# Expert stage: gathered rows transposed by VectorE instead of TensorE, and gathered three tiles ahead

## The chip, the cores and the metric

One Trainium2 chip, one core. The metric is the device time of one execution in microseconds (us), median over runs. Engines: PE is TensorE, DVE VectorE, ACT ScalarE, POOL GpSimd, SP SyncE.

## What is computed

Three layers follow one another: linear attention on 8 x 8 heads of 576 positions, a gated dense layer, and a layer of 8 experts. In the reference, cut to what matters here (N = 4608 tokens, D = 512, F = 1024, E = 8):

```python
logits = x @ w_gate
expert_idx = np.argmax(logits, axis=1)
gate_w = softmax(logits)[np.arange(N), expert_idx]
for e in range(E):
    mask = expert_idx == e
    xe = x[mask]
    h = np.maximum(xe @ w1[e], 0.0)
    ye = h @ w2[e]
    out[mask] = gate_w[mask, None] * ye
```

## The kernel before

The program is written engine by engine; each engine runs its own list in order, with waits on semaphores. A fp32 operand of a matmul is kept as two parts, `hi` (rounded) and `lo` (the rest), and a product is the sum of three matmuls (`split3`). So each operand costs a cast (ScalarE) and a subtraction (VectorE).

The expert stage works on tiles of 128 tokens of one expert. With these inputs there are 40 tiles, g = 0 to 39. Tiles 0 to 2 (`FIRST` = 3) and the last are written out; tiles 3 to 38 are a loop on every engine (`tiles`), whose bounds and addresses come from a table in memory (`table`). One pass of the loop for tile g is, engine by engine:

- PE (`tile`, L1763): `first_product(g)`, two halves of 12 matmuls of 512 columns; `x_transpose(g + 1)`, four transposes of 128 x 128 from the gathered rows `xg` into the PSUM bank `xtr_ps` (L1715); `second_product(g - 2)`, 24 matmuls.
- ACT (L1288): `relu_stored(g)` from PSUM to `hs` (L1257); `rows_high(g + 1)`, the cast from `xtr_ps` to the high half of `xt` (L1232); `next_gate` (L1242); `turned_h_high(g - 1)`, the cast of `hturn` to the high half of `ht` (L1286); then the casts of the weight chunks that the table gives to this tile (L810).
- DVE (L1504): `rows_low(g + 1)`, the subtraction from `xtr_ps` for the low half of `xt` (L1463); `turn_h(g - 1)`, one transpose of 128 x 1024 in blocks of 32 x 32 from `hq` to `hturn` (L1489); `result(g - 2)`, PSUM to `ysb` (L1470); `turned_h_low(g - 1)`, the subtraction for the low half of `ht` (L1494); the subtractions of the weight chunks (L1501).
- POOL (`period`): `gather(g + 2)`, an indirect DMA of 128 rows of 513 numbers into `xg` (L1086), with the gate of the tile before saved first (L1077); `scatter(g - 2)`, an indirect DMA of `ysb` to the output (L1109).
- SP (L1025): `store_rows(g)`, h to memory; `load_quarters(g)`, h back into `hq` with its quarters exchanged, so that 32 x 32 blocks complete its transpose; `loads_of(g - 1)`, loads of weight chunks of 1 MB into four slots (`ahead`).

An expert's weights are four chunks of 128 x 2048. They lie split in `ring`, which holds two experts; the table says at which tile each chunk is cast.

`hturn` is the low half of `ht`, so `turn_h(g - 1)` waits for the end of the second product of the tile before, and `turned_h_low` subtracts in place. There is one `xt` buffer, one `xg`, one `hq` and one `ysb`. In the loop `xt` is written between two first products:

```python
def x_transpose(g):
    pe.wait_ge(gathered, 16 * g + 16)
    for c in range(DC):
        last = pe.transpose(xtr_ps[:, c * P:(c + 1) * P], xg[:, c * P:(c + 1) * P], m["ident"][:])
    last.then_inc(xtr_mm, 1)
```

Of the kernel before, what the change touches and what calls it, by code (L numbers as in the profile page):

```python
# [22 lines left out]
F32 = mybir.dt.float32  # L23
# [43 lines left out]
def alloc(nc, ctx):  # L67
# [58 lines left out]
    for name, n, dt in (("ident", P, F32), ("tri", P, F32), ("ones", P, F32),   # L126
                        ("wgate", DC * E, F32), ("absmax", 8 * PT, F32), ("cden", H * S // DK, F32),
                        ("ibase", BQ * E, F32), ("idesc", BQ * E, F32),
                        ("cum", (BQ + 1) * E, F32), ("rt", 4 * BQ * E, F32), ("lg", BQ * E, F32), ("rq", 6 * BQ, F32),
                        ("slot", BQ, U32), ("tokf", BQ, F32),  # L130
                        ("ids0f", FIRST, F32), ("ids0", FIRST, U32), ("pad", 2, F32),
                        ("idall", 3 * P, U32), ("idg", 1, U32), ("ids", 1, U32),
                        ("gate", 1, F32), ("gnext", 1, F32), ("tabf", 5 * GMAX, F32), ("tab", 5 * GMAX, I32),
                        ("thr", E * TPE, F32), ("gi", GMAX * E, F32), ("nte", 4 * E, F32),
                        ("lowtri", E * E, F32)):
        m[name] = sb(name, [P, n], dt)
# [690 lines left out]
def stage2(nc, m, t):  # L827

    with ExitStack() as ctx:
# [18 lines left out]
        h_turned, gate_saved = sem("s3_h_turned"), sem("s3_gate_saved")  # L848
        h_stored, hq_in = sem("s3_h_stored"), sem("s3_hq_in")
# [195 lines left out]
        def _(pool):  # L1045
# [43 lines left out]
            def gather(g):  # L1089
                if isinstance(g, int):  # L1090
                    pool.wait_ge(gate_set, g)
                    pool.wait_ge(xtr_mm, g)
                    ids_of(g)
                else:
                    keep_gate(g - 1)
                    ids_of(g)
                    pool.wait_ge(gate_saved, g)
                    pool.wait_ge(xtr_mm, g)
                gather_rows(g)
# [39 lines left out]
            gather(FIRST + 1)  # L1139
            pool.wait_ge(y_sb, 2)  # L1140
# [4 lines left out]
            def period(g):  # L1145
                gather(g + 2)
                scatter(g - 2)

            last = tiles(pool, period, 2)
# [15 lines left out]
        def _(act):  # L1165
# [71 lines left out]

            def next_gate(g):
                for h in range(2):
                    act.wait_ge(relu_done[h], g)  # L1240
                act.wait_ge(gate_saved, g + 1)
                act.copy(m["gate"][:], m["gnext"][:]).then_inc(gate_set, 1)  # L1242
# [45 lines left out]
            def tile(g):  # L1288
                relu_stored(g)
                rows_high(g + 1, False)  # L1290
                next_gate(g + 1)
                turned_h_high(g - 1)
                tile_chunks(act, g, weights)
# [28 lines left out]
        def _(dve):  # L1322
# [142 lines left out]

            def result(g):
# [37 lines left out]
            def tile(g):  # L1504
                rows_low(g + 1)
                turn_h(g - 1)
                result(g - 2)
                turned_h_low(g - 1)
                tile_chunks(dve, g, weights)

            dve.sem_inc(h_turned, 2)
            turns(dve, turn)
# [44 lines left out]
            dve.tensor_copy(m["idall"][:], last_ps[:, 0:3 * P]).then_inc(idt_sb, 1)  # L1557
# [49 lines left out]
            linked(dve.tensor_scalar_add(tabf[:, 3, 4:5], tabf[:, 3, 0:1], -4.0), base)  # L1607
            dve.tensor_copy(m["tab"][:, 0:ROW], m["tabf"][:, 0:ROW]).then_inc(tabs, 1)
# [8 lines left out]
            weights(CPE)  # L1617
            weights(CPE + 1)
            last = tiles(dve, tile)
            last1 = last_of(dve, 1)  # L1620
# [10 lines left out]
        def _(pe):  # L1631
# [131 lines left out]
            def tile(g):  # L1763
# [3 lines left out]
                x_transpose(g + 1)  # L1767
# [90 lines left out]
```

## Time and profile before

| | |
|---|---|
| median of 3 runs | 1505.48 us (1502.93 to 1506.18) |
| the profiled execution | 1503.65 us, span of its core 1501.9 us |
| TensorE busy | 1470.3 us |
| VectorE busy | 877.1 us |
| ScalarE busy | 620.6 us |
| GpSimd busy | 527.4 us |
| granted TensorE clock | 0.995 of full speed |

The last third of the span, from about 1040 us on, is the loop over tiles and its end. How to read the rows: in a timeline each row has the start in us from the span's start, the length in us, the engine, the line of the kernel, the operation, what it writes and reads, how many were merged, and in brackets how long the engine had been idle before it and what ended that. Lines are those of the kernel before; L167 is the helper that records every split matmul.

### The profile page before, as it was taken

The numbers are of one execution on the slowest core, as the hardware profiler recorded it, in microseconds if no ns is written. First come the engines' busy times: TensorE is split into PE (matmuls) and PEld (weight loads), VectorE is DVE, ScalarE is ACT, GpSimd is POOL, SyncE is SP. The second block draws the span as 40 slices with busy tenths as digits, with TensorE's granted clock in tenths as the row PEclk, the third lists the DMA queues.
The fourth block names the chain that finished last, engine by engine and source line by source line (L and its number), as shares of the span: only waits on it lengthen the run. The fifth ranks groups of instructions, "written<-read, shape, count | busy, mean of one in ns | idle before, by whom it ended". The sixth has DMA issues, their size and how long they took to land.

```text
span 1501.9 us, 29607 instructions
## 1 busy us (share of the span) xinstructions
PE 1470.3 (98%) x8062; PEld 1272.5 (85%) x8063; DVE 877.1 (58%) x1629; ACT 620.6 (41%) x1295; POOL 527.4 (35%) x653
## 2 busy tenths in 40 slices
PE   7999999999989999999999999999999999999996
PEld 6999999999978888888888888888888778888885
DVE  4688888888825473746547274635555545553332
ACT  5688788788822122221212222133344334442221
POOL 6676677676820020120202022030344333332321
PEclk9999999999999999999999999999999999999999
DMA  7354344444440112020211202065676767653441
GB/s 259 111 140 102 103 112 102 111 104 114 120 129 0 41 44 83 1 84 4 79 35 49 78 6 84 2 152 147 217 233 221 236 211 230 229 193 132 140 142 40
DMA packets 111242, 173.49 MB, mean 116 GB/s; under 512 B 52976, under 2 KB 72176, under 8 KB 106978
## 3 DMA queue, kind: packets, MB, share of 16 engines
q1 hardware_dynamic: 103618, 152.82, 34.2%
q0 software_dynamic: 7584, 20.17, 4.0%
q8 instruction: 21, 0.34, 0.1%
q14 instruction: 19, 0.16, 0.0%
HBM read 123.66 MB, written 50.34 MB: 116 GB/s over the span
## 4 chain that ended last, share of the span: by engine, by line
PE 68%; DMA 1%; issue 1%; DVE 1%; SPq 0%; ACT 0%; ACTq 0%; POOL 0%; POOLq 0%; DVEq 0%
PE bank L167 66%; PE bank L1715 1%; DMA h_scratch<-arena 0%; DMA arena<-we 0%; DMA arena<-rows_scratch,idg 0%; PE bank L1646 0%; SPq L1022 0%; DMA arena<-h_scratch 0%; PE bank L1759 0%; DVE hturn L1489 0%; DVE big L1501 0%; PE bank L1654 0%; PE bank L1665 0%; ACT big L810 0%; PE bank L1640 0%
## 5 line engine op out<-in xcount | busy, mean ns | idle before, releaser
L167 PE MATMUL bank<-big,xs 128*128 (+1 forms) x2100 | 493.5, 393 | 13.2 <-DVE big L610 8.1
L167 PEld LDWEIGHTS bank<-big,xs 128*128 128x128 f32 x2100 | 392.4, 189 | 95.2 <-issue 14.7
L167 PE MATMUL bank<-xs,big 128*128 128x512 f32 x1728 | 397.4, 391 | 2.7 <-PEq L216 2.7
L167 PEld LDWEIGHTS bank<-xs,big 128*128 128x128 f32 x1728 | 324.7, 188 | 70.4 <-issue 3.0
L167 PE MATMUL bank<-big 128*128 128x512 f32 (+1 forms) x1632 | 325.9, 348 | 2.0 <-POOL big L306 1.4
L167 PEld LDWEIGHTS bank<-big 128*128 128x128 f32 (+1 forms) x1632 | 255.9, 165 | 36.2 <-POOL big L306 1.7
L1050 POOL TENSOR_TENSOR arena<-arena 128x512 f32<-128x512 f32 x32 | 41.0, 1293 | 438.2 <-DMA arena<-rec_scratch 438.2
L1432 DVE TENSOR_TENSOR arena<-arena,bank 128x512 f32<-128x512 f32 x72 | 49.5, 687 | 243.9 <-PE bank L167 243.9
L1189 ACT COPY arena<-bank 128x512 f32<-128x512 f32 x72 | 42.4, 589 | 307.0 <-PE bank L167 307.0
L1357 DVE CUSTOM_DVE_ANT_0 arena<-arena 128x512 f32<-128x512 f32 x256 | 159.6, 689 | 16.1 <-ACT arena L1209 15.4
L704 PE MATMUL bank<-arena 128*128 128x66 f32 (+1 forms) x1152 | 147.8, 269 | 0.0
L704 PEld LDWEIGHTS bank<-arena 128*128 128x128 f32 x1152 | 142.3, 191 | 0.2
L1109 POOL DMA_INDIRECT out<-arena,ids x38 | 69.0, 1815 | 209.1 <-DVE arena L1470 202.1
L181 POOL TENSOR_TENSOR kqs<-kqraw,kqs 128x256 fp32r<-128x256 f32 (+1 forms) x160 | 128.2, 801 | 12.8
L508 ACT ACTIVATE arena<-arena 128x256 f32<-128x256 f32 (+1 forms) x320 | 110.4, 399 | 50.9 <-DVE arena L634 40.8
L167 PE MATMUL bank<-wphis,kqs 128*128 128x256 f32 x864 | 130.8, 290 | 0.3
L1286 ACT CAST xs<-hturn 128x1024 fp32r<-128x1024 f32 x37 | 39.0, 1053 | 191.2 <-DVE hturn L1489 191.2
L622 DVE TENSOR_REDUCE absmax<-bank 128x4 f32<-128x512 f32 (+1 forms) x160 | 100.7, 630 | 22.2 <-PE bank L167 21.6
L634 DVE TENSOR_TENSOR arena<-bank,absmax 128x512 f32<-128x512 f32 (+1 forms) x160 | 102.2, 639 | 18.0
L167 PEld LDWEIGHTS bank<-wphis,kqs 128*128 128x128 f32 x864 | 111.3, 189 | 1.7 <-DVE arena L634 1.5
L1489 DVE STREAM_TRANSPOSE hturn<-arena 128x1024 f32<-128x1024 f32 x37 | 46.1, 1245 | 106.1 <-PE bank L167 96.7
L1501 DVE TENSOR_TENSOR big<-arena,big (+1 forms) x28 | 64.1, 2295 | 52.4 <-ACT big L810 52.4
(182 smaller groups left out, 1350.6 us busy)
## 6 DMA issues: line engine op xcount, KB each, us to landing
arena<-we SPq DMA_DIRECT2D x32, 1024.0 KB, 11.5
h_scratch<-arena SPq DMA_DIRECT2D x37, 512.0 KB
arena<-h_scratch SPq DMA_DIRECT2D x148, 128.0 KB
kqraw<-kq SPq DMA_DIRECT2D x32, 576.0 KB, 3.8
rows_scratch<-arena SPq DMA_DIRECT2D x36, 256.5 KB
xT_scratch<-arena SPq DMA_DIRECT2D x32, 288.0 KB
arena<-v SPq DMA_DIRECT2D x64, 128.0 KB, 2.4
arena<-xT_scratch SPq DMA_DIRECT2D x8, 1024.0 KB, 5.2
```

Source lines behind the costliest of these rows:

```text
L167: ins = nc.tensor.matmul(out, left[a], right[b], start=first and n == 0, stop=last and n == 2)
L181: pool.tensor_tensor(m["kqs"][:, 1, u, cols], m["kqraw"][:, u, cols], m["kqs"][:, 0, u, cols].bitcast(F32), ALU.subtract).then_inc(m["kq_l ...
L508: last = act.activation(ke[:, rows[0]:rows[-1] + 1, s * P:(s + 1) * P], pm[:, rows[0]:rows[-1] + 1, 0], ACT.Exp, scale=1.0 - 2.0 * s)
L622: dve.tensor_reduce(absmax[:, bank, 0:n], proj_ps[bank][:, 0:2 * n * P].rearrange("p (t a f) -> p t a f", t=n, a=2), AX.X, ALU.max, apply_ ...
L634: dve.tensor_tensor(pm[:, rows[0]:rows[-1] + 1], proj_ps[bank][:, 0:2 * n * P].rearrange("p (t a f) -> p t a f", t=n, a=2), absmax[:, bank ...
L704: last = pe.matmul(kv_ps[:, s, cols[0]:cols[1]], ke[:, r, s * P:(s + 1) * P], v[:, u, slots[0]:slots[1]].rearrange("p t d -> p (t d)"), st ...
L1109: pool.indirect_dma_start(t["out"], bass.IndirectOffsetOnAxis(m["ids"][:, 0:1], 0), ysb, None, bounds_check=N - 1, oob_is_err=False).then_ ...
L1189: act.copy(asb[:, j % 2], a_ps[j % 2][:]).then_inc(a_sb, 1)
L1357: dve.tensor_tensor_reduce(products[e % 2], x2[:, q, 0:DM], m["wgrows"][:, e * DM:(e + 1) * DM], 1.0, 0.0, ALU.mult, ALU.add, lg[:, n:n + ...
L1432: dve.tensor_tensor(abf[:, j % 2], asb[:, j % 2], b_ps[j % 2][:], ALU.mult).then_inc(ab_f, 1)
L1489: dve.transpose(m["hturn"].rearrange("p (k b j) -> p k b j", k=FC, b=P // Q), hq.rearrange("p (b k i) -> p k b i", b=P // Q, k=FC)).then_i ...
L1501: dve.tensor_tensor(ring[:, 1, ds(at, CW)], ahead[:, ds(slot, CW)], ring[:, 0, ds(at, CW)].bitcast(F32), ALU.subtract).then_inc(w_lo, 1)
```

## The change

The transposes of the gathered rows leave TensorE from tile 4 on. VectorE does them instead (`turn_rows`), from `xg` to a new buffer `xturn`. Its transpose works on blocks of 32 x 32 within 32 partitions, so 128 x 128 is put together from sixteen instructions a tile: for each quarter a of the partitions written and each quarter b of those read, one transposes four blocks, 32 partitions by 128 elements. The cast and the subtraction for `xt` then read `xturn` instead of PSUM (`turned_rows_high`, `turned_rows_low`).

`turn_rows(g + 2)` stands in VectorE's pass for tile g, after the subtraction for tile g + 1 and ahead of `turn_h(g - 1)`. `xg` is free when it is done, so GpSimd's gather runs three tiles ahead instead of two, and waits for VectorE (`x_turned`) instead of TensorE. Ahead of the loop, VectorE turns tile 4 between the two weight chunks that stand there, and GpSimd gathers tile 5. The end of the loop is written out for one tile more on VectorE and GpSimd, the table gets one more entry, and the list of tokens `idall` is cut to the 288 columns in use.

```diff
+                        ("xturn", DM, F32), ("idall", E * TPE + 4, U32), ("idg", 1, U32), ("ids", 1, U32),
...
             def gather(g):
-                if isinstance(g, int):
+                if isinstance(g, int) and g <= FIRST + 1:
                     pool.wait_ge(gate_set, g)
                     pool.wait_ge(xtr_mm, g)
                     ids_of(g)
@@
                     keep_gate(g - 1)
                     ids_of(g)
                     pool.wait_ge(gate_saved, g)
-                    pool.wait_ge(xtr_mm, g)
+                    pool.wait_ge(x_turned, g)
                 gather_rows(g)
@@
             gather(FIRST)
             gather(FIRST + 1)
+            gather(FIRST + 2)
...
             def period(g):
-                gather(g + 2)
+                gather(g + 3)
                 scatter(g - 2)
@@
+            def turned_rows_high(g):
+                act.wait_ge(x_turned, g + 1)
+                act.wait_ge(h_mm, 2 * g)
+                act.copy(m["xt"][:, 0], m["xturn"][:]).then_inc(xt_hi, 1)
@@
             def tile(g):
                 relu_stored(g)
-                rows_high(g + 1, False)
+                turned_rows_high(g + 1)
                 next_gate(g + 1)
                 turned_h_high(g - 1)
                 tile_chunks(act, g, weights)
@@
+            def turn_rows(g):
+
+                dve.wait_ge(xt_lo, g)
+                dve.wait_ge(gathered, 16 * g + 16)
+                by_token = xg[:, 0:DM].rearrange("p (c a j) -> p a c j", c=DC, a=P // Q)
+                by_row = m["xturn"][:].rearrange("p (c b i) -> p b c i", c=DC, b=P // Q)
+                for a in range(P // Q):
+                    for b in range(P // Q):
+                        last = dve.transpose(by_row[a * Q:(a + 1) * Q, b], by_token[b * Q:(b + 1) * Q, a])
+                last.then_inc(x_turned, 1)
+
+            def turned_rows_low(g):
+                dve.wait_ge(xt_hi, g + 1)
+                dve.wait_ge(h_mm, 2 * g)
+                dve.tensor_tensor(m["xt"][:, 1], m["xturn"][:], m["xt"][:, 0].bitcast(F32), ALU.subtract
+                                  ).then_inc(xt_lo, 1)
@@
             def tile(g):
-                rows_low(g + 1)
+                turned_rows_low(g + 1)
+                turn_rows(g + 2)
                 turn_h(g - 1)
                 result(g - 2)
                 turned_h_low(g - 1)
                 tile_chunks(dve, g, weights)
 
             dve.sem_inc(h_turned, 2)
+            dve.sem_inc(x_turned, FIRST + 1)
...
             weights(CPE)
+            turn_rows(FIRST + 1)
             weights(CPE + 1)
-            last = tiles(dve, tile)
-            last1 = last_of(dve, 1)
+            last = tiles(dve, tile, 2)
...
@@
                 for h in range(2):
                     first_product(g, h, *here)
-                x_transpose(g + 1)
                 second_product(g - 2, *before)
```

How the instructions of the loop stand on VectorE, from the instruction ahead of the loop to the first half of a pass. `arena` is the memory that holds `xg`, `hq` and `ysb`; `xs` holds `xt` and `ht`; `big` is `ring`. Before:

```order
L1501 TENSOR_TENSOR big<-arena,big 128x2048 x2
L824 TENSOR_LOAD tab
L824 ISA x2
L915 UNCONDITIONAL_BRANCH
L915 ISA
L1463 TENSOR_TENSOR xs<-bank,xs 128x512
L1487 ISA
L1489 STREAM_TRANSPOSE hturn<-arena 128x1024
L1469 ISA
L1470 COPY arena<-bank 128x512
L1493 ISA
L1494 TENSOR_TENSOR xs<-hturn,xs 128x1024
```

And in the change:

```order
L1482 STREAM_TRANSPOSE xturn<-arena 32x4x32 x16
L1526 TENSOR_TENSOR big<-arena,big 128x2048
L824 TENSOR_LOAD tab
L824 ISA x2
L916 UNCONDITIONAL_BRANCH
L916 ISA
L1487 ISA
L1488 TENSOR_TENSOR xs<-xturn,xs 128x512
L1477 ISA
L1482 STREAM_TRANSPOSE xturn<-arena 32x4x32 x16
L1512 ISA
L1514 STREAM_TRANSPOSE hturn<-arena 128x1024
```

Sixteen transposes stand between the subtraction for `xt` and the transpose of h in each pass, with no wait among them (ISA rows are waits and register work), and another sixteen between the two weight chunks ahead of the loop.

On TensorE, between the first and the second product of a pass. Before:

```order
L167 MATMUL bank<-big,xs 128x512 x2
L1713 ISA
L1715 MATMUL bank<-ident,arena 128x128 x4
L1732 REGISTER_ALU
L1737 ISA
```

And in the change:

```order
L167 MATMUL bank<-big,xs 128x512
L167 ISA
L167 MATMUL bank<-big,xs 128x512 x2
L1766 REGISTER_ALU
L1771 ISA
```

The four transposes and their wait for the gather are gone; the second product follows the first at once.

## Rows read from the trace of the kernel before

**Rows 1.** The page's table of engines: busy us, share of the span, instructions

```profile
PE 1470.3 (98%) x8062; PEld 1272.5 (85%) x8063; DVE 877.1 (58%) x1629; ACT 620.6 (41%) x1295; POOL 527.4 (35%) x653
```

**Rows 2.** The chain of waits in the loop: start us, us, what

```profile
1302.36 0.44 PE bank L1715 x4
1302.80 10.92 PE bank L167 x48
```

**Rows 3.** Groups of instructions on TensorE, whole span: busy us, mean ns, idle before

```profile
L1715 PE MATMUL bank<-ident,arena 128*128 128x128 f32 x160 | 24.0, 273 | 0.1
```

**Rows 4.** VectorE's timeline, one tile with one chunk

```profile
1297.03 1.25 DVE L1489 STREAM_TRANSPOSE hturn<-arena 128x1024 f32<-128x1024 f32 x1 [3.11 <-PE bank L167]
...
1299.51 1.23 DVE L1494 TENSOR_TENSOR xs<-hturn,xs 128x1024 fp32r<-128x1024 f32 x1 [0.67 <-ACT xs L1286]
...
1302.38 2.29 DVE L1501 TENSOR_TENSOR big<-arena,big  x1 [1.64 <-ACT big L810]
...
1304.59 0.68 DVE L1463 TENSOR_TENSOR xs<-bank,xs 128x512 fp32r<-128x512 f32 x1
...
1308.38 1.25 DVE L1489 STREAM_TRANSPOSE hturn<-arena 128x1024 f32<-128x1024 f32 x1 [3.10 <-PE bank L167]
```

**Rows 5.** Groups of instructions on VectorE, 1060 to 1475 us

```profile
L1494 DVE TENSOR_TENSOR xs<-hturn,xs 128x1024 fp32r<-128x1024 f32 x36 | 44.1, 1226 | 24.0 <-ACT xs L1286 24.0
L1463 DVE TENSOR_TENSOR xs<-bank,xs 128x512 fp32r<-128x512 f32 x36 | 24.7, 687 | 39.5 <-ACT xs L1232 38.8 <-issue 0.7
```

**Rows 6.** VectorE's timeline, two instructions with no wait between

```profile
1033.48 0.28 DVE L1547 TENSOR_SCALAR arena<-arena,rq 128x128 f32<-128x128 f32 x1
1033.67 0.43 DVE L1548 TENSOR_SCALAR arena<-arena,rq 128x288 f32<-128x288 f32 x1
```

**Rows 7.** VectorE's timeline, the two memsets of 64 partitions

```profile
2.44 0.17 DVE L594 MEMSET arena<- 64x132 f32 x1
2.69 0.17 DVE L595 MEMSET arena<- 64x132 f32 x1
```

**Rows 8.** VectorE's timeline, two instructions linked by a semaphore

```profile
1047.82 0.15 DVE L1604 TENSOR_SCALAR tabf<-tabf 128x1 f32<-128x1 f32 x1
1048.01 0.15 DVE L1605 TENSOR_SCALAR tabf<-tabf 128x1 f32<-128x1 f32 x1
```

**Rows 9.** ScalarE's timeline in the same tile as rows 4

```profile
1298.36 1.05 ACT L1286 CAST xs<-hturn 128x1024 fp32r<-128x1024 f32 x1 [5.71 <-DVE hturn L1489]
...
1300.08 1.91 ACT L810 CAST big<-arena  x1 [0.67 <-issue]
...
1301.89 1.26 ACT L1257 ACTIVATE arena<-bank,gate 128x512 f32<-128x512 f32 x2
```

**Rows 10.** Groups of instructions on VectorE, 1060 to 1475 us: the weight chunks

```profile
L1501 DVE TENSOR_TENSOR big<-arena,big x26 | 59.6, 2296 | 52.4 <-ACT big L810 52.4
```

**Rows 11.** VectorE's timeline, first transpose of h, and first after the last chunk

```profile
1064.55 1.25 DVE L1489 STREAM_TRANSPOSE hturn<-arena 128x1024 f32<-128x1024 f32 x1 [3.82 <-PE bank L167]
...
1365.20 1.25 DVE L1489 STREAM_TRANSPOSE hturn<-arena 128x1024 f32<-128x1024 f32 x1 [3.11 <-PE bank L167]
```

**Rows 12.** A tile without a chunk: a piece of the chain, and VectorE's timeline

```profile
1381.90 0.44 PE bank L1715 x4
...
1383.43 0.69 DVE L1463 TENSOR_TENSOR xs<-bank,xs 128x512 fp32r<-128x512 f32 x1 [3.16 <-ACT xs L1232]
```

**Rows 13.** Ahead of the loop: a piece of the chain, and timelines

```profile
1045.16 3.60 DMA arena<-rows_scratch,idg
...
1051.74 0.97 POOL L1086 DMA_INDIRECT arena<-rows_scratch,idg  x1 [0.83 <-DVE arena L1470]
...
1053.74 4.48 DVE L1501 TENSOR_TENSOR big<-arena,big 128x2048 fp32r<-128x2048 f32 x2
...
1057.36 0.91 POOL L1077 COPY gnext<-arena 128x1 f32<-128x1 f32 x1 [3.30 <-DMA arena<-rows_scratch,idg]
```

**Rows 14.** VectorE's timeline, a chunk in one of the first ten tiles

```profile
1105.16 2.29 DVE L1501 TENSOR_TENSOR big<-arena,big  x1 [2.82 <-ACT big L810]
```

More of the change, by code:

```diff
@@ L131, in alloc @@
                         ("ids0f", FIRST, F32), ("ids0", FIRST, U32), ("pad", 2, F32),
-                        ("idall", 3 * P, U32), ("idg", 1, U32), ("ids", 1, U32),
+                        ("xturn", DM, F32), ("idall", E * TPE + 4, U32), ("idg", 1, U32), ("ids", 1, U32),
                         ("gate", 1, F32), ("gnext", 1, F32), ("tabf", 5 * GMAX, F32), ("tab", 5 * GMAX, I32),
@@ L848, in stage2 @@
         h_turned, gate_saved = sem("s3_h_turned"), sem("s3_gate_saved")
+        x_turned = sem("s3_x_turned")
         h_stored, hq_in = sem("s3_h_stored"), sem("s3_hq_in")
@@ L1145, in period @@
             def period(g):
-                gather(g + 2)
+                gather(g + 3)
                 scatter(g - 2)
-            last = tiles(pool, period, 2)
+            last = tiles(pool, period, 3)
+            scatter(last_of(pool, 4))
             keep_gate(last)
@@ L1556, in _ @@
             dve.wait_ge(idt_mm, 1)
-            dve.tensor_copy(m["idall"][:], last_ps[:, 0:3 * P]).then_inc(idt_sb, 1)
+            dve.tensor_copy(m["idall"][:, 0:E * TPE], last_ps[:, 0:E * TPE]).then_inc(idt_sb, 1)
             linked(dve.tensor_tensor(gw, gi, ends.unsqueeze(1).to_broadcast([P, GMAX, E]), ALU.is_ge), base)
@@ L1607, in _ @@
             linked(dve.tensor_scalar_add(tabf[:, 3, 4:5], tabf[:, 3, 0:1], -4.0), base)
+            linked(dve.tensor_scalar_add(tabf[:, 3, 5:6], tabf[:, 3, 0:1], -5.0), base)
             dve.tensor_copy(m["tab"][:, 0:ROW], m["tabf"][:, 0:ROW]).then_inc(tabs, 1)
@@ L1617, in _ @@
             weights(CPE)
+            turn_rows(FIRST + 1)
             weights(CPE + 1)
-            last = tiles(dve, tile)
-            last1 = last_of(dve, 1)
+            last = tiles(dve, tile, 2)
+            last1, last2 = last_of(dve, 1), last_of(dve, 2)
+            turned_rows_low(last)
+            turn_h(last2)
+            result(last_of(dve, 3))
+            turned_h_low(last2)
+            tile_chunks(dve, last1, weights)
             last_low()
```

## The prediction

> **What bounds the kernel now.** I read the page's table of engines first: TensorE is busy for 98% of the span, VectorE for 58% [rows 1]. Then the chain of waits in the expert stage: it is TensorE alone, 10.93 us for 48 matmuls, then 0.44 us for the four transposes of the gathered rows, 11.37 us a tile [rows 2]. So the transposes lie on the path. The groups of instructions give their number: 160 records for 40 tiles, 24.0 us busy, 0.15 us each when overlapped [rows 3]; four of the 40 sets (tiles 0 to 3) stay. Last I read VectorE's timeline of one tile, since the work goes there [rows 4]: transpose of h (1297.03), result copy, subtraction for `ht`, weight chunk (1302.38), subtraction for `xt` (1304.59), and then 3.10 us of waiting for TensorE before the next transpose of h at 1308.38. That idle time is all that VectorE can take on in such a tile before it sets the pace.
>
> **What goes.** 36 sets of transposes on TensorE, 36 x 0.44 = 15.8 us of the chain. If TensorE stayed the bound everywhere, that would be the result: about 1488 us. ScalarE's and VectorE's `xt` steps read SBUF in place of PSUM; VectorE takes 1226 ns for 1024 columns from SBUF and 687 ns for 512 from PSUM [rows 5], one price per column, so I cost this at nothing; the reads stand on the path only where VectorE does, and are counted there.
>
> **What comes: sixteen transposes a tile on VectorE.** One covers 32 partitions and 128 elements each. Its length: the rows of 512 and 1024 columns differ by 539 ns, 1.05 ns a column [rows 5]; the transpose of 1024 columns takes 1.25 us [rows 4], so 0.17 us is fixed, and 128 columns take 0.17 + 0.13 = 0.30 to 0.31 us. What decides is the distance from one start to the next, and the trace of before has no such series. Its bounds:
> - Below: two instructions with no wait between, all on partitions from 0 up, overlap. The compare of 128 columns at 1033.48 lasts 0.28 us and the next starts 0.19 us after it [rows 6]. At 0.19 to 0.20 us sixteen take 3.0 to 3.2 us.
> - Above: the only pair without a wait whose partitions change is that of the two memsets of 64 rows (partitions 64 to 127, then 0 to 63). They do not overlap: 0.17 us long, 0.25 us apart [rows 7], 0.08 us from end to start. At 0.31 + 0.08 = 0.39 us sixteen take 6.2 us.
> - Between: where each instruction waits for the one before by a semaphore, the start comes 0.04 us after the end (0.15 us long, 0.19 apart) [rows 8].
>
> In the change the quarter that is read differs from one transpose to the next in all sixteen, so the memsets are the nearest pair: I take no overlap. For the gap I take the 0.04 us of instructions that read, since a memset reads nothing: 0.31 + 0.04 = 0.35 us, R = 5.6 us a tile. Bounds 5.0 (no gap) to 6.2.
>
> The memsets show a change of the partitions written, not of those read. Taken that narrowly, only the four transposes that begin a new output quarter would be serial, and the sum 1522 (third rival). The Trainium skill, "VectorE: DVE Perf Modes", section on two Vector instructions with no wait between them, says that one is held until all earlier ones have finished when its first input or its output starts in another group of 32 partitions than the last. By it all sixteen are held and the sum is the one below, 1571. No row here shows a changed input alone. The same page, section on the three transpose paths, gives 311 ns for a VectorE transpose of 128 columns and says that it stays within 32 x 32 blocks, so TensorE is its choice for a full one; by its figure the sixteen would be an estimated 5.0 us plus gaps.
>
> **A tile with one weight chunk.** VectorE's own chain: from the transpose of h to the chunk 5.35 us (1297.03 to 1302.38), chunk to `xt` subtraction 2.21, that one 0.68 and 0.04 to the sixteen, which wait for it, then R, then the next transpose of h [rows 4]. The 5.35 us can't shrink, because the chunk's cast on ScalarE (1300.08, 1.91 us) stands behind its cast of the turned h (1298.36) [rows 9]. Sum 8.28 + 5.6 = 13.88 us, against 11.35 now. TensorE needs 10.93 and idles 2.9 us in each.
>
> Queued behind the sixteen on VectorE: `turn_h`, `result`, `turned_h_low`, the chunk. The second product waits for `turned_h_low`, SyncE's quarter loads and weight loads for `turn_h`, GpSimd's scatter for `result`. These come late together and stay in the same order; the scatter and the loads have the longer tile to finish in.
>
> **The run of tiles.** In the loop there are 26 chunks [rows 10]; the timeline has them as 10 tiles with one, one with two, one with none, 14 with one, then 10 tiles with none. From the first transpose of h in the loop to the first after the last chunk now: 1064.55 to 1365.20, 300.65 us for 26 tiles [rows 11]. Changed: 24 x 13.88 = 333.1. The tile with two chunks takes one more 2.2: 16.1. The one without: ScalarE's cast of the turned h ends 2.4 us after the transpose of h began; then it has its table loads, two activations (1.26 us together) and the cast for `xt` [rows 9], so I estimate that the `xt` subtraction starts at 5.4, and the tile takes 5.4 + 0.7 + 5.6 = 11.7. Sum 360.9: **+60.3 us**.
>
> **The start.** VectorE turns tile 4 between two chunks ahead of the loop. Now the two run together, 4.48 us from 1053.74; the rows of tile 4 are gathered from 1051.74 on and are there at 1057.36, when GpSimd's copy that waited for them starts [rows 13]. So turning is 1057.4 to 1063.0, the chunk to 1065.2, the `xt` subtraction to 1065.9. The gather for tile 5 now waits for the first turning: from about 1063.1, with 3.6 us (the gather at 1045.16 was in the chain for that long) to 5.6 us, to 1066.7; turning to 1072.3. The transpose of h stood at 1064.55: **+7.7**.
>
> **The end.** At the last chunk TensorE is no longer 5.9 us from its next second product when `turn_h` starts, but 3.7, since the first product is done: **-2.2**. In the ten tiles without chunks the `xt` subtraction starts 1.5 us after the first product's end (1383.43, and the chain goes over to the transposes at 1381.90) [rows 12]; 1.5 + 0.7 + 5.6 + 3.7 (transpose of h to the end of the `ht` subtraction [rows 4]) = 11.5 where TensorE wants it at 10.93. A second product that starts 0.6 late gives the next tile as much room, so they take 11.2 on average, against 11.37: **-1.5**.
>
> **First ten tiles.** There ScalarE reaches its chunk up to 1 us later (VectorE waits 2.82 us for it at 1105.16, against 1.64 at 1302.38 [rows 4, 14]), while DMA is fullest. Now TensorE hides it, then nothing would: 0 to +10. DMA has a fifth more time in the longer tile; I take **+3**.
>
> **Sum:** 60.3 + 7.7 - 2.2 - 1.5 + 3 = +67.3. The profiled execution took 1503.65 us (span 1501.9), inside the runs' 1502.93 to 1506.18 and 1.8 below their median. Forecast **1571 us**. The 15.8 us are all given back, and four times as much again.
>
> **Range of this case.** R = 5.0 is 0.6 x 26 = 16 less and 2 less at the start and the end; with nothing for the first ten tiles 1550. R = 6.2 gives 16 more and 4 at the start and the end; with the whole +10, 1598. A gather that is late would also be dear: issued at the end of one turning, it is needed 13.88 - 5.6 = 8.3 us later, and takes 3.6 to 5.6 [rows 13]; at 9 it would add 0.7 x 26 = 18 us, 1589. Range 1549 to 1600, a step beyond both ends.
>
> **Rivals.**
> 1. *The transposes overlap* (faster, 8%). Place: the same sixteen instructions. The point from which it decides is a pitch of (11.35 - 8.28) / 16 = 0.19 us, and the compares show just that. Against: the memsets, and the compares never move between partitions. At 0.19: R = 3.0, a tile with a chunk takes 11.3 as now; the last ten are TensorE's at 10.93, 4.4 less; the waits of TensorE about the tile with two chunks shrink by at most 2: **1497**. At 0.20 to 0.21, or with the first ten tiles' cost, it is a tie.
> 2. *TensorE stays the bound in all tiles* (faster, 1%): 1488. It needs R below 10.93 - 8.28 = 2.65, a pitch of 0.17.
> 3. *Only a new output quarter is serial* (slower, 7%). Four at 0.35 and twelve at 0.20: R = 3.8, a tile 12.08: 24 x 0.73 = 17.5 more; start +4, first ten +3, the end -2.2 - 4.4: **1522**. For it: the memsets show no more. Against: nothing shows an input moved without cost.
> 4. *Serial, as forecast* (slower, 84%).
>
> A change within 0.2% (3 us, about what can be told from none) lies about a pitch of 0.19 to 0.20. Of the first rival's 8%, 4 are faster by more than that, 3 the tie, 1 slower. Faster 4 + 1 = 5%, same 3%, slower 84 + 7 + 1 = 92%. The range of the forecast's own case holds nearly all of its 84%, so it stands.
>
> **What would show it.** In the changed profile: transposes of `xturn` with starts 0.35 us apart and 5.6 us in all; the group of L1715's transposes with 16 records; tiles of 13.9 us between transposes of h up to the last chunk, with TensorE waiting 2.9 us ahead of each second product for the `ht` subtraction; tiles of about 11.2 after it; the chain of waits on VectorE for most of the expert stage. Starts 0.2 us apart would make it wrong at the root; starts 0.35 apart with tiles near 11.4 would mean that the 5.35 us before the chunk shrinks after all.

## The result, and the profile after

The changed kernel took **1562.82 us** (median of 4 runs, 1559.56 to 1563.42), the kernel before 1505.83 on the same chip (4 runs, 1502.93 to 1507.56): a ratio of 1.0376, interval 1.0354 to 1.0398. The forecast was 1571, range 1549 to 1600. The profiled execution took 1563.42 us, span 1561.7, so the span grew by 59.8 us.

The page's table of engines for the changed kernel:

```profile
PE 1481.9 (95%) x7918; PEld 1270.4 (81%) x7919; DVE 1057.2 (68%) x2206; ACT 619.6 (40%) x1295; POOL 497.9 (32%) x653
```

TensorE has 144 matmuls fewer than in [rows 1], 36 sets of four, and is nevertheless busy 11.6 us longer (the last section returns to this). VectorE has 577 instructions and 180.1 us more, of which the page's group of transposes holds 576 and 174.5 us (busy us, mean ns; then idle time ahead):

```profile
L1482 DVE STREAM_TRANSPOSE xturn<-arena 32x128 f32<-32x128 f32 x576 | 174.5, 303 | 16.3 <-DMA arena<-rows_scratch,idg 4.2
```

The chain of waits in the same stage, at the start of one set of sixteen (start us, us, what):

```profile
1313.48 0.30 DVE xturn L1482
1313.79 0.01 issue
1313.80 0.30 DVE xturn L1482
...
1314.11 0.30 DVE xturn L1482
1314.41 0.01 issue
1314.42 0.30 DVE xturn L1482
```

Starts 0.31 us apart, 0.01 us from end to start, one strictly after the other. And they stand in the chain, where [rows 2] had nothing but TensorE. VectorE's timeline of one tile with a chunk, to be laid beside [rows 4]:

```profile
1332.05 1.25 DVE L1514 STREAM_TRANSPOSE hturn<-arena 128x1024 f32<-128x1024 f32 x1
1333.22 0.65 DVE L1495 COPY arena<-bank 128x512 f32<-128x512 f32 x1
1334.54 1.22 DVE L1519 TENSOR_TENSOR xs<-hturn,xs 128x1024 fp32r<-128x1024 f32 x1 [0.66 <-ACT xs L1294]
1337.41 2.29 DVE L1526 TENSOR_TENSOR big<-arena,big  x1 [1.65 <-ACT big L810]
1339.62 0.68 DVE L1488 TENSOR_TENSOR xs<-xturn,xs 128x512 fp32r<-128x512 f32 x1
1340.44 5.05 DVE L1482 STREAM_TRANSPOSE xturn<-arena 32x128 f32<-32x128 f32 x16
1345.53 1.25 DVE L1514 STREAM_TRANSPOSE hturn<-arena 128x1024 f32<-128x1024 f32 x1
```

The 3.1 us in which VectorE waited for TensorE are gone. 5.36 us from the transpose of h to the chunk, as before; the sixteen take 5.09 us up to the next transpose of h; the tile 13.48. TensorE's timeline around the same place:

```profile
1322.48 11.19 PE L167 MATMUL bank<-big,xs 128*128 x48 [0.69 <-DVE xs L1519]
1335.96 12.77 PE L167 MATMUL bank<-big,xs 128*128 x48 [2.29 <-DVE xs L1519]
1349.44 11.17 PE L167 MATMUL bank<-big,xs 128*128 x48 [0.70 <-DVE xs L1519]
```

Each row is a tile's second product and the first product behind it. So in every tile TensorE now waits ahead of the second product for VectorE's subtraction for `ht`, 0.7 and 2.3 us by turns. Where the span's 59.8 us lie:

| stretch | before, us | after, us | difference | forecast |
|---|---|---|---|---|
| up to the first transpose of h in the loop | 1064.55 | 1073.55 | +9.0 | +7.7 |
| from there to the first one after the last chunk | 300.65 | 352.84 | +52.2 | +63.3 |
| the rest | 136.7 | 135.3 | -1.4 | -3.7 |

The rows are those of one execution. The first stretch differs from one to the next: in *swapped* below, with the same sixteen instructions there, it ends at 1069.66, since the first turning finds its rows already there. The stretch ends so (VectorE's timeline of the changed kernel):

```profile
1057.87 5.05 DVE L1482 STREAM_TRANSPOSE xturn<-arena 32x128 f32<-32x128 f32 x16 [1.55 <-DMA arena<-rows_scratch,idg]
1062.95 2.29 DVE L1526 TENSOR_TENSOR big<-arena,big 128x2048 fp32r<-128x2048 f32 x1
1065.16 0.68 DVE L1488 TENSOR_TENSOR xs<-xturn,xs 128x512 fp32r<-128x512 f32 x1
1068.47 5.05 DVE L1482 STREAM_TRANSPOSE xturn<-arena 32x128 f32<-32x128 f32 x16 [2.63 <-DMA arena<-rows_scratch,idg]
1073.55 1.25 DVE L1514 STREAM_TRANSPOSE hturn<-arena 128x1024 f32<-128x1024 f32 x1
```

and one of the last ten tiles, without a chunk, looks so: VectorE,

```profile
1460.53 1.25 DVE L1514 STREAM_TRANSPOSE hturn<-arena 128x1024 f32<-128x1024 f32 x1
...
1466.00 0.69 DVE L1488 TENSOR_TENSOR xs<-xturn,xs 128x512 fp32r<-128x512 f32 x1 [1.75 <-ACT xs L1244]
1466.84 5.05 DVE L1482 STREAM_TRANSPOSE xturn<-arena 32x128 f32<-32x128 f32 x16
1471.92 1.25 DVE L1514 STREAM_TRANSPOSE hturn<-arena 128x1024 f32<-128x1024 f32 x1
```

and ScalarE:

```profile
1461.87 1.05 ACT L1294 CAST xs<-hturn 128x1024 fp32r<-128x1024 f32 x1 [7.29 <-DVE hturn L1514]
1463.79 1.27 ACT L1265 ACTIVATE arena<-bank,gate 128x512 f32<-128x512 f32 x2 [0.87 <-issue]
1465.24 0.62 ACT L1244 CAST xs<-xturn 128x512 fp32r<-128x512 f32 x1 [0.18 <-ACT arena L1265]
```

Here TensorE sets nothing. The tile is a loop of VectorE and ScalarE: transpose of h, its cast, the table loads (0.87), two activations, the cast for `xt`, its subtraction (5.47 us after the transpose of h began), the sixteen. It takes 11.39 us, as long as the tile before the change. Eight of the ten tiles are such, 11.36 to 11.40. The ninth takes 9.77: its pass has no rows left to turn. That tile, 1.6 us shorter than before, is the -1.4 of the table's last line; the tenth takes 11.80, before 11.81.

### The profile page after: what moved, and what is told of

The parts are those of the page before. It is cut to its first block and busy times, and to the rows that moved or that the text cites. A ratio compares the mean times of both kernels' runs of the same rounds, so it can differ in the third digit from the quotient of the medians.

```text
span 1561.7 us, 29935 instructions
## 1 busy us (share of the span) xinstructions
PE 1481.9 (95%) x7918; PEld 1270.4 (81%) x7919; DVE 1057.2 (68%) x2206; ACT 619.6 (40%) x1295; POOL 497.9 (32%) x653
## 5 line engine op out<-in xcount | busy, mean ns | idle before, releaser
L167 PE MATMUL bank<-big,xs 128*128 (+1 forms) x2100 | 510.7, 403 | 61.9 <-DVE xs L1519 50.2
L167 PEld LDWEIGHTS bank<-big,xs 128*128 128x128 f32 x2100 | 405.7, 195 | 162.4 <-issue 77.8
L1482 DVE STREAM_TRANSPOSE xturn<-arena 32x128 f32<-32x128 f32 x576 | 174.5, 303 | 16.3 <-DMA arena<-rows_scratch,idg 4.2
L1087 POOL DMA_INDIRECT arena<-rows_scratch,idg x37 | 38.1, 1030 | 203.9 <-DVE xturn L1482 202.2
L1526 DVE TENSOR_TENSOR big<-arena,big (+1 forms) x28 | 64.1, 2292 | 43.6 <-ACT big L810 43.6
## 6 DMA issues: line engine op xcount, KB each, us to landing
arena<-we SPq DMA_DIRECT2D x32, 1024.0 KB, 11.7
```

The lines of the kernel that those rows point to most:

```text
L167: ins = nc.tensor.matmul(out, left[a], right[b], start=first and n == 0, stop=last and n == 2)
L1482: last = dve.transpose(by_row[a * Q:(a + 1) * Q, b], by_token[b * Q:(b + 1) * Q, a])
L1526: dve.tensor_tensor(ring[:, 1, ds(at, CW)], ahead[:, ds(slot, CW)], ring[:, 0, ds(at, CW)].bitcast(F32), ALU.subtract).then_inc(w_lo, 1)
```

## Experiments

All change the changed kernel, by the diff shown. A single run's time is set beside the kernel before on the same chip: 1506.51 us for the first four, 1502.93 for *late*, *behind_chunk* and *moved*, 1505.07 for *late_scatter* and *behind_scatter*, 1504.14 for *moved_act*, 1505.28 for *chunk_first*. "Tile" is the distance between transposes of h in tiles with one chunk.

### What sets the pitch of the sixteen

**same_quarter.** Each transpose reads the quarter that it writes, so 12 of 16 change neither (its blocks off the diagonal are other data than the reference's).

```diff
-                        last = dve.transpose(by_row[a * Q:(a + 1) * Q, b], by_token[b * Q:(b + 1) * Q, a])
+                        last = dve.transpose(by_row[a * Q:(a + 1) * Q, b], by_token[a * Q:(a + 1) * Q, b])
```

> The sixteen transposes stay, but in each group of four both the quarter read and the quarter written stay the same (the turned rows are then not the transposed ones: blocks outside the diagonal are wrong, so h and the output are). Theory (a transpose waits for the end of the one before only when its partitions move): inside a group the starts are 0.19 to 0.21 us apart, between groups 0.32; R = 12 x 0.20 + 4 x 0.32 = 3.7 us, a tile with a chunk 8.40 + 3.7 = 12.1 us, the time about 1518 us. Rival (transposes never overlap, wherever they read and write): all starts 0.32 apart, R = 5.1, 13.5 us a tile, 1562 us.

Measured 1517.67 us, tile 12.0. The chain of waits shows groups of four:

```profile
1309.00 0.88 DVE xturn L1482 x4
1309.88 0.01 issue
1309.89 0.88 DVE xturn L1482 x4
```

Within a group there are three pitches of 0.19 us and one whole instruction; between groups there is a gap of 0.01 us and no overlap. The same sixteen instructions of the same size take 3.6 us instead of 5.08. The pitch is a matter of quarters, not of the transpose.

**swapped.** The loops over a and b exchange places: 12 of 16 change only the quarter written, where the changed kernel has 12 that change only the quarter read.

```diff
-                for a in range(P // Q):
-                    for b in range(P // Q):
+                for b in range(P // Q):
+                    for a in range(P // Q):
```

> The two loops exchanged: the quarter written changes with each transpose, the quarter read with every fourth. Nothing else changes. Theory (a change of either is enough): starts 0.32 us apart, 1562 us within 3. Rival (only one of the two counts, and the other's cost is what the changed kernel paid): starts 0.20 apart inside a group, about 1518 us.

Measured 1558.66 us (one run, 3.3 below the 1562 expected; it comes to the loop's first transpose of h 3.9 us sooner than the changed kernel), tile 13.47, starts 0.31 to 0.32 apart. Either change, of the quarter read or of the one written, holds the instruction. With the changed kernel's own rows this ends the third rival.

**twelve and eight.** Fewer transposes: `for a in range(3)` and `for a in range(2)`. The rest of `xturn` is zero, so a quarter or a half of each gathered row's transpose is left out.

```diff
-                for a in range(P // Q):
+                for a in range(3):
@@
-            dve.sem_inc(x_turned, FIRST + 1)
+            dve.memset(m["xturn"][:], 0.0).then_inc(x_turned, 1)
+            dve.wait_ge(x_turned, 1)
+            dve.sem_inc(x_turned, FIRST)
```

> Twelve of the sixteen transposes, the last quarter of xturn left at zero (a quarter of the contraction is left out in tiles from 4 on). Theory (VectorE's own chain, 8.40 us and the transposes, sets the tile): R = 3.8, a tile with a chunk 12.2 us, tiles without one 10.93, the time 1562.8 - 26 x 1.27 - 2.5 - 4.4 = about 1523 us. Rival (the gather, which now waits for VectorE and takes some 5.5 us to land, or GpSimd's queue sets it): less than half of that is won, over 1540.

> Eight of the sixteen, half of xturn left at zero (half of the contraction is left out in tiles from 4 on). Theory: R = 2.5, 8.40 + 2.5 = 10.9, so TensorE sets the pace again at 10.93 us a tile and the whole gain of its lost transposes shows, but for the start: about 1489 us. Rival (a slow TensorE clock after each wait, or the gather, keeps tiles at 11.2 or more): 1497 or more.

Twelve: 1527.25 us, tile 12.3, most of the last ten 10.88. Eight: 1497.25 us, tile 10.93 in most from the seventh on. Four transposes are worth 1.2 us a tile while VectorE sets the pace, and with eight the pace is TensorE's. Both came out longer than expected. Twelve missed by 4 us, in two tiles: 13.62 near the start and 15.2 behind the tile without a chunk. Eight missed by 8 us and came out at its rival's 1497, but not for the rival's reason: its usual tile is 10.93 and not 11.2, and the granted clock fell only once in the loop. Its first six tiles take 11.2 to 11.9, since ScalarE comes late to its chunk there (3 us in all), and the three tiles about the one with two chunks take 13.36, 9.74 and 15.76, 6 us more than three of 10.93. In the longest of them ScalarE's activations wait 5.22 us for the store of h.

### Where the sixteen stand

VectorE still waits 0.66 + 1.65 us a tile for ScalarE ahead of the `ht` subtraction and the chunk. Could the sixteen fill that?

**late.** Behind the `ht` subtraction, ahead of the chunk.

```diff
             def tile(g):
                 turned_rows_low(g + 1)
-                turn_rows(g + 2)
                 turn_h(g - 1)
                 result(g - 2)
                 turned_h_low(g - 1)
+                turn_rows(g + 2)
                 tile_chunks(dve, g, weights)
```

> turn_rows(g + 2) moved behind turned_h_low(g - 1), ahead of the weight chunk, where VectorE now idles 1.65 us for ScalarE's cast. Theory (VectorE's chain is its work plus its waits for ScalarE, and work put into a wait is free): from the transpose of h 3.75 us to the sixteen, 5.08, the chunk 2.21, the xt subtraction 0.60: 11.7 us a tile with a chunk, the tiles without one 10.9, the start 7 us earlier; about 1505 us in all, no change against the kernel before. Rival (VectorE is simply 5.1 us fuller, wherever they stand, or the gather behind them comes late): 13.4 us a tile, over 1550.

Measured **1626.23 us** (1620.84 to 1630.37), ratio 1.0804 (1.0772 to 1.0837). The theory fell. VectorE's timeline, then GpSimd's:

```profile
1342.92 0.69 DVE L1495 COPY arena<-bank 128x512 f32<-128x512 f32 x1 [3.24 <-DMA out<-arena,ids]
...
1344.66 5.04 DVE L1482 STREAM_TRANSPOSE xturn<-arena 32x128 f32<-32x128 f32 x16
```

```profile
1350.69 2.80 POOL L1087 DMA_INDIRECT arena<-rows_scratch,idg  x1 [8.75 <-DVE xturn L1482]
...
1354.66 1.03 POOL L1110 DMA_INDIRECT out<-arena,ids  x1 [0.97 <-POOL ids L1106]
```

GpSimd's queue has the scatter behind the gather three tiles ahead, and that gather waits for the sixteen. Turned later, they hold the gather, the gather holds the scatter, and the next result copy on VectorE waits for the scatter that frees `ysb`: 3.24 us here. I had counted who waits for the sixteen, and not who stands behind the one that waits.

**behind_chunk.** Behind the chunk too, last in the pass.

```diff
                 turned_h_low(g - 1)
                 tile_chunks(dve, g, weights)
+                turn_rows(g + 2)
```

> The sixteen behind the weight chunk, so no longer ahead of turn_h and the ht subtraction, but not in a wait either. Theory (what counts is the sum round the loop): 8.3 + 5.1 = 13.4 us a tile with a chunk, about 1555 us. Rival (the harm is that the transposes delay turn_h and with it the second product; anywhere behind it they are free): about 11.4 us a tile, 1505 us.

Measured 1681.12 us, one run, most tiles 16.9 to 17.8; in one of them the result copy waits 5.51 us for the scatter.

**late_scatter and behind_scatter.** The same two, with GpSimd's scatter ahead of its gather.

```diff
             def period(g):
-                gather(g + 3)
                 scatter(g - 2)
+                gather(g + 3)
```

> The run with the sixteen ahead of the chunk again, with GpSimd's scatter(g - 2) now ahead of its gather(g + 3). Theory (in that run the scatter stood behind a gather that waited for the sixteen, and VectorE's result copy waited for the scatter, a circle of two engines; and of VectorE's 1.65 us ahead of the chunk about 1 us is its own table loads, which only a wait can hide): the result copy waits no more, 3.75 + 5.08 + 1.05 + 2.21 + 0.6 = 12.7 us a tile with a chunk, 10.9 without, about 1533 us. Rival (the gather that comes late is what costs): the tiles stay at 14 us or more, over 1570.

> The run with the sixteen behind the chunk again, with the scatter ahead of the gather. Theory (sum round VectorE's loop): 5.35 + 2.21 + 5.08, then 0.87 of waiting for ScalarE's cast of the turned rows, which can now start only behind the sixteen, and 0.60: 14.1 us a tile with a chunk, about 1570 us. Rival (harm only ahead of turn_h): 11.4 us a tile, 1505.

late_scatter: **1536.14 us** (1534.84 to 1546.15), ratio 1.0228 (1.0193 to 1.0263), tile 12.1 in most after the first five. The whole came out near what was expected (1533), but its parts didn't: the tile was to be 12.7, of which the table loads ahead of the chunk took 0.6 instead of 1.05, and the first five tiles took 13.0 to 14.7. behind_scatter: 1570.11 us, one run, tile 14.10. One exchange of two calls on GpSimd takes 90 and 111 us off, so the loop through the scatter is shown. It also shows what the place is worth: ahead of the chunk the sixteen run while ScalarE casts it, the tile is 1.4 us shorter than the changed kernel's 13.47 and the whole 27 us; behind the chunk there is no wait to fill, and a new one comes: the `xt` subtraction waits 0.87 us for ScalarE's cast of rows that were turned only just before.

**moved.** GpSimd copies the gathered rows to a second buffer `xh` as soon as they and the last turning are done, so the next gather waits for that copy and not for VectorE. Two transposes stand ahead of the `ht` subtraction, fourteen ahead of the chunk.

```diff
+            def move_rows(g):
+                pool.wait_ge(x_turned, g)
+                pool.sem_inc(turn_taken, 1)
+                pool.tensor_copy(m["xh"], xg[:, 0:DM]).then_inc(x_moved, 1)
@@
-                    pool.wait_ge(x_turned, g)
+                    move_rows(g - 1)
+                    pool.wait_ge(x_moved, g)
@@
                 turned_rows_low(g + 1)
-                turn_rows(g + 2)
                 turn_h(g - 1)
                 result(g - 2)
+                turn_rows(g + 2, 0, 2)
                 turned_h_low(g - 1)
+                turn_rows(g + 2, 2, 16)
                 tile_chunks(dve, g, weights)
```

> GpSimd first copies the gathered rows to a second buffer (128 x 512, estimated at 1.2 to 1.7 us from its 128 x 256 and 128 x 512 rows), from which VectorE turns them, and gathers the next at once, so the sixteen may be spread: two in VectorE's wait of 0.66 us for the cast of the turned h, fourteen ahead of the chunk. Theory: both waits are filled, 11.0 to 11.1 us a tile with a chunk, 10.9 without, about 1496 us, faster than both kernels. Rival (GpSimd and VectorE slow each other, or the copy comes late): 11.5 us a tile or more, 1505 or more.

Measured **1518.97 us** (1517.30 to 1522.34), ratio 1.0105 (1.0085 to 1.0125), 44 us below the changed kernel. Tiles 11.6 to 12.0. What was missing against the expectation stands ahead of the chunk in VectorE's timeline:

```profile
1301.95 0.59 DVE L1492 STREAM_TRANSPOSE xturn<-xh 32x128 f32<-32x128 f32 x2
...
1303.95 4.43 DVE L1492 STREAM_TRANSPOSE xturn<-xh 32x128 f32<-32x128 f32 x14
1309.42 2.29 DVE L1537 TENSOR_TENSOR big<-arena,big  x1 [1.05 <-issue]
```

1.05 us in which VectorE waits for nobody: the reading of the table with the chunk's place, 0.6 to 1.6 us in this run, 0.9 on average. It was always there, inside the 1.65 us of waiting for ScalarE. A wait that is filled with work doesn't come back whole. The time lies where the rival put it, but the rival's reason isn't in the trace: VectorE waits for GpSimd nowhere in the tiles, its instructions are as long as before (2.29, 1.23 and a pitch of 0.32), and GpSimd's copy takes 0.61 us. What makes the reading 0.6 us in one tile and 1.05 in another isn't shown.

**moved_act.** As moved, the loop's result copy on ScalarE, four transposes in the first gap and twelve in the second.

```diff
+            def act_result(g):
+                act.wait_ge(y_mm, g + 1)
+                act.wait_ge(scattered, 16 * g)
+                act.copy(ysb, y_ps[:]).then_inc(y_sb, 1)
@@
                 turned_h_high(g - 1)
+                act_result(g - 2)
                 tile_chunks(act, g, weights)
@@
                 turned_rows_low(g + 1)
-                turn_rows(g + 2)
                 turn_h(g - 1)
-                result(g - 2)
+                turn_rows(g + 2, 0, 4)
                 turned_h_low(g - 1)
+                turn_rows(g + 2, 4, 16)
```

> The kernel in which GpSimd copies the gathered rows first, with the result copy (PSUM to ysb) moved from VectorE to ScalarE in the loop, and four instead of two of the sixteen in VectorE's wait ahead of the ht subtraction. Theory (in that kernel VectorE has no wait left but 1 us of table loads and sets the tile at 12.0 us by its work alone): 0.65 us of work less gives 11.35 us a tile with a chunk and 10.9 without, about 1500 us, just ahead of the kernel before. Rival (the copy on ScalarE delays its casts, or the two last waits on PSUM and the output come back): 12 us or more, 1515 or more.

Measured **1502.30 us** (12 runs, 1498.13 to 1504.34) against 1504.14 (17 runs), ratio 0.9988 (0.9977 to 0.9998). That is 0.12%, less than the 0.2% that can be told from no change. Most tiles with a chunk take 11.0 to 11.7, most of the last ten 10.88. So the idea of the change can be brought to a tie with the kernel before, by filling every gap of VectorE and taking one copy from it; no version that computes the whole reference was clearly faster. A way to exchange the quarters outside VectorE, so that one transpose of 128 x 512 would do, wasn't tried.

### The gather that landed late at the start

**chunk_first.** In the changed kernel the rows of tile 5 landed 5.5 us after the turning of tile 4 ended. Here the weight chunk stands ahead of that turning.

```diff
             weights(CPE)
-            turn_rows(FIRST + 1)
             weights(CPE + 1)
+            turn_rows(FIRST + 1)
```

> The one place where the start went otherwise than forecast: the gather for tile 5 landed 5.5 us after the turning of tile 4 ended. In the changed kernel GpSimd takes 2.34 us for this gather (from 1063.74) and 1.00 us for nearly all others, and while it does, VectorE runs the weight chunk's subtraction (1062.95, 2.29 us), which reads two operands in SBUF; in the kernel before the gathers beside such a chunk take 2.6 to 2.9 us and end 0.87 us after the chunk does, the others 1.00. Here that chunk stands ahead of the turning instead of behind it, so that only the subtraction for xt (0.68 us) is beside the gather. Theory A (VectorE's subtraction from two SBUF operands keeps GpSimd from working on the gather): GpSimd takes 1.0 to 1.4 us for it, the rows land about 4.1 us after the turning's end, and the first transpose of h comes within 0.2 us of where it is now relative to a turning that starts about 0.7 us later, near 1072.9 against 1073.55. Theory B (the gather is slow because GpSimd or the queue is cold, or because of DMA load): it takes 2.3 us again, the rows land 5.5 us after the turning, the first transpose of h near 1074.3. The whole time stays within a microsecond of the changed kernel's, too little for one run to tell; the trace decides.

GpSimd's timeline, in the changed kernel:

```profile
1063.74 2.34 POOL L1087 DMA_INDIRECT arena<-rows_scratch,idg  x1 [4.97 <-DVE xturn L1482]
```

and in this one:

```profile
1062.96 0.97 POOL L1087 DMA_INDIRECT arena<-rows_scratch,idg  x1 [5.75 <-DVE xturn L1482]
```

0.97 us instead of 2.34, and VectorE begins to turn tile 5 at 1066.33, 4.2 us after the turning ended at 1062.13: theory A. From the first turning to the transpose of h it is 14.32 us instead of 15.68; by theory A it was to be 14.3. (The turning itself began 0.8 us earlier than in the changed kernel, where I had expected it later: in this run all that stands ahead of it came some 1.2 us sooner. So the differences are to be compared, not the stamps.) The whole took 1561.03 us, one run; that this order is faster isn't shown.

## Why the prediction was right, and where it was off

**The step on which all rested held.** All sixteen run one after the other, both when only the quarter read changes and when only the one written does (changed kernel, *swapped*), and they overlap when neither does (*same_quarter*, at the 0.19 us of [rows 6]). By the rule of the Trainium skill, "VectorE: DVE Perf Modes", section on two Vector instructions with no wait between them, that was to come; this case's traces agree, with 0.31 to 0.32 us against 0.19. The first and third rivals fall with it, the second too.

**The pitch was mis-sized, 0.35 for 0.317.** 0.04 us of gap was taken from [rows 8]; the gap is 0.01, and the length 303 ns. I gave an instruction that waits for no semaphore the gap of one that does; it starts sooner. R was 5.08, near the lower bound of 5.0; in 24 tiles that is 12.5 us less. (The 311 ns that the Trainium skill gives in "VectorE: DVE Perf Modes", section on the three transpose paths, stand there for 128 x 128 numbers in bf16, not for fp32 pieces of 32 x 128.)

**A tile with a chunk:** 13.88 forecast, 13.47 measured. The 5.35 us ahead of the chunk didn't shrink, as said. The other terms were 0.1 short (0.14 us from the `xt` subtraction to the sixteen, where I had 0.04), 2.5 us in 24 tiles. That the reads of SBUF in place of PSUM cost nothing held: the `xt` subtraction takes 0.68 us as before.

**The two odd tiles:** 16.1 and 11.7 forecast, 15.68 and 11.42 measured. What I hadn't seen is the tile behind them, 14.80. VectorE waits 2.97 us for its chunk there instead of 1.65, because ScalarE's cast of it waits 1.99 us for the weights to land, where it otherwise spends 0.68 on its own table loads: +1.3. SyncE, which had two weight loads in a row there, also sent the store of h late, but ScalarE's activations waited only 0.23 us for that. (In *eight* it is that store on which the same tile waits.)

**First ten tiles:** +3 taken, of which one tile at 14.35 (ScalarE's cast waits 1.55 us for the weights) and one at 13.57 show, +1. TensorE did hide ScalarE's lateness before, but in the longer tile ScalarE is no longer late: VectorE waits 43.6 us for 25 chunks, 1.7 each, so nearly everywhere as in the tile above.

**The run:** 363.9 forecast with these +3, 352.84 measured: -10 for the 24 tiles with one chunk (the pitch less the 0.1), -0.7 for the odd tiles, +1.3 for the one behind them, -2 for the first ten.

**The start:** +7.7 forecast, +9.0 measured. Turning began 0.5 later and each set was 0.5 shorter; the rows were there 5.5 us after the turning's end, where I had used 0.1 + 3.6 and had written up to 5.6. Of the 1.8 us between them 0.7 is that GpSimd starts the gather 0.82 us after the turning's end. *chunk_first* shows the larger part: the chunk's subtraction that I had put behind the turning stood beside the gather, which took GpSimd 1.37 us longer by it. Both operands of that step were in my text, their meeting was not.

**The last ten tiles:** 11.2 on average forecast, 11.36 to 11.40 measured in eight of them; with the -2.2 for the last chunk -3.7 forecast for the rest, -1.4 measured. The failed step is "a second product that starts 0.6 late gives the next tile as much room". It supposes that the loop goes through TensorE. The rows above show that it doesn't; it is VectorE's and ScalarE's, 5.47 + 0.84 + 5.08, and nothing catches up in it. For the same reason the -2.2 never came: the first tile behind the last chunk takes 11.40 like the others. What did come, the ninth tile's 9.77, wasn't in the sum. That the loop comes to the old 11.37 is chance: with twelve and with eight transposes most of the same tiles take TensorE's 10.88.

In sum +59.8 us of span for +67.3: the largest part of the miss is the pitch, and that the other terms nearly cancel is luck. The first rival's 1497 had a slip: it leaves out the start, which by the same working is +2.5 at R = 3.0, so about 1500, a tie. The sign and the size came from one question, whether neighbours overlap, answered from the memsets of [rows 7] rather than from the many overlapping pairs.

## What to carry to other kernels

Before many short instructions are put on an engine, price the distance between their starts and not their length: find in the trace a pair that changes partitions as they would (0.19 us or more than 0.3 here, which put the forecasts 74 us apart). When a step is moved, follow the queue of each engine that waits for it to the instructions behind the waiting one: two calls exchanged on GpSimd, which is busy 32% of the changed kernel's span, were worth 90 us in *late*. And a gap in which an engine waits for another also hides its own register and table work; read that from a place where it isn't covered before counting the gap as free.

## What the runs showed that I had not expected

**VectorE's subtraction of a weight chunk holds back a gather of GpSimd's that starts behind it.** GpSimd takes 1.00 us for a gather, but 2.94 for the one at 1105.38 in the kernel before, in the tile of [rows 14]:

```profile
1105.38 2.94 POOL L1086 DMA_INDIRECT arena<-rows_scratch,idg  x1 [1.82 <-DMA out<-arena,ids]
```

The chunk that began at 1105.16 ended at 1107.45, and the gather 0.87 us later. The same distance follows for the gather at the start of the changed kernel (chunk to 1065.24, gather to 1066.08: 0.84) and in *late* (1352.62 and 1353.49: 0.87). In the changed kernel every later gather of the loop starts beside the transpose of h, and takes 0.99 to 1.00 us. The Trainium skill, "SBUF — State Buffer", section on SBUF's two separate sides, says that VectorE with two SBUF inputs and a GpSimd instruction that reads SBUF share a pair of ports, which whichever starts first holds for its whole instruction. The trace agrees as far as the gather is the later one: 0.97 us where the chunk was moved away and 2.34 where it wasn't.

What decides is indeed which of the two starts first. These gathers stood beside a chunk too, one in the kernel before (its chunk began at 1082.75) and one in *late* (chunk at 1321.15):

```profile
1082.66 0.99 POOL L1086 DMA_INDIRECT arena<-rows_scratch,idg  x1 [1.83 <-PE bank L1715]
1320.81 1.00 POOL L1087 DMA_INDIRECT arena<-rows_scratch,idg  x1 [9.62 <-DVE xturn L1482]
```

They began 0.09 and 0.34 us ahead of the chunk and were not held; GpSimd's short copy behind the first of them, begun beside the chunk, was (1.39 us for 0.20). Nor did the gathers hold the chunk, which took 2.29 us as it does alone. By the Trainium skill's rule it would have been blocked; in that direction the rule isn't borne out here. What in the gather reads SBUF isn't shown.

**TensorE's clock fell after most of its longer waits.** The timeline of the kernel before has the 48 matmuls of [rows 2] so:

```profile
1302.55 11.17 PE L167 MATMUL bank<-big,xs 128*128 x48
```

(The chain's 10.92 us counts from the end of the transposes, which they overlap.) In the changed kernel they take 11.19 and 12.77 by turns. The trace in windows of 1 us over the longer one (window; us; busy PE, PEld, DVE, ACT, POOL with counts; granted clock; DMA share; GB/s):

```profile
1336.00:1337.00 1.00, 1.00 (x4) 0.84 (x5) 0.00 (x0) 1.00 (x2) 0.66 (x1) 0.76 0.96 297
1337.00:1338.00 1.00, 1.00 (x4) 0.81 (x3) 0.59 (x1) 1.00 (x3) 0.00 (x0) 0.50 1.06 306
1338.00:1339.00 1.00, 1.00 (x4) 0.81 (x3) 1.00 (x1) 0.82 (x3) 0.00 (x0) 0.50 0.97 258
1339.00:1340.00 1.00, 1.00 (x4) 0.72 (x3) 1.00 (x2) 0.07 (x1) 0.41 (x1) 0.54 0.95 287
1340.00:1341.00 1.00, 1.00 (x6) 0.83 (x5) 0.85 (x3) 0.00 (x0) 0.26 (x1) 1.00 0.86 279
```

After TensorE had waited 2.29 us (to 1335.96), the granted clock fell to 0.50, the level of 1.2 GHz, for some 3.4 us, and then returned to 2.4 GHz. The 48 matmuls took 1.60 us longer by it. In the 26 tiles of the run this happened 11 times, in ten of them for about as long and once, from 1104 to 1111, for 7 us; together it added some 19 us of busy time. It happened after waits of 2.28 to 5.59 us, and after none of those near 0.7. But after five long waits the clock stayed at 1.00 (2.27 us to 1145.81, 2.89 to 1228.86 and 2.29 to 1430.30 among them); what decides isn't shown. That is how TensorE, rid of 144 transposes, is busy 11.6 us longer: a tile had 11.36 us of its work without a gap and has 11.18 at the full clock now, 6.5 us less in 36 tiles, and the low clock adds the 19 (12.5 more by these two, 11.6 measured). It cost nothing here, since VectorE sets the pace: 12.77 + 0.70 and 11.19 + 2.29 are the same tile. I had written 10.93 us of work and 2.9 of waiting for each.
